# Sinkhorn routing inside an attention-and-experts kernel: partition sums by all-ones matmuls on TensorE in place of GpSimd's reduce

## What is computed

```python
x = window_attention(q, k, v)              # 4 x 8 heads, 576 positions, width 64, window 64 -> [2304, 512]
logits = x @ w_gate                        # [2304, 8]
P = np.exp(logits - logits.max())
for _ in range(8):
    P /= P.sum(1, keepdims=True) + 1e-09   # sums over the 8 experts
    P /= P.sum(0, keepdims=True) + 1e-09   # sums over all 2304 tokens
    P *= N / E
for e in range(8):
    out += P[:, e:e + 1] * (np.maximum(x @ w1[e], 0.0) @ w2[e])
```

## Time and profile before

| | us |
|---|---|
| median of 3 executions (lowest to highest) | 1751.09 (1749.76 to 1754.01) |
| the profiled execution, its own time | 1752.63 |
| its span in the trace | 1750.8 |
| PE busy | 1633.5 |
| POOL busy | 998.6 |
| DVE busy | 725.3 |
| ACT busy | 525.8 |

### The profile page before, as it was taken

One profiled execution on the slowest core, in us unless ns is written; L12 is line 12 of the kernel. 1 busy time (PEld: TensorE's weight loads), 2 busy tenths in 40 slices (PEclk: granted clock), 3 DMA queues, 4 the chain that ended last, 5 costly groups with the idle time before them and its releaser, 6 DMA issues.

```text
span 1750.8 us, 23864 instructions
## 1 busy us (share of the span) xinstructions
PE 1633.5 (93%) x8652; PEld 1465.1 (84%) x8652; DVE 725.3 (41%) x1260; ACT 525.8 (30%) x751; POOL 998.6 (57%) x654
## 2 busy tenths in 40 slices
PE   6878453999999999999999999999999999999999
PEld 6777342888888888898888888898888888898888
DVE  4563212444344344344434434434433443443443
ACT  2332001323333233432333323333333332333332
POOL 5662121666555667766655566567865556655562
PEclk8988775999999999999999999999999999999999
DMA  7841000221122211132112221121311121112210
GB/s 224 239 132 41 8 24 24 72 73 72 48 72 72 72 68 52 72 109 73 64 56 72 72 72 60 60 72 72 108 57 64 72 72 72 52 68 72 72 60 36
DMA packets 35432, 129.17 MB, mean 74 GB/s; under 512 B 4288, under 2 KB 4416, under 8 KB 35392
## 3 DMA queue, kind: packets, MB, share of 16 engines
q1 hardware_dynamic: 35392, 128.65, 21.5%
HBM read 123.91 MB, written 4.72 MB: 73 GB/s over the span
## 4 chain that ended last, share of the span: by engine, by line
PE 85%; issue 7%; DMA 3%; POOL 2%; DVE 1%; SPq 0%; ACT 0%; POOLq 0%; DVEq 0%
PE ps L393 15%; PE ps L394 15%; PE ps L392 15%; PE ps L376 13%; PE ps L372 13%; PE ps L374 13%; DMA qk_buf<-qk 3%; PE ps L289 1%; POOL w_lo L602 1%; PE ps L310 1%; POOL w_lo L609 1%; PE ps L320 1%; DVE xv_lo L751 0%; DVE p_t L730 0%; PE ps L300 0%
## 5 line engine op out<-in xcount | busy, mean ns | idle before, releaser
L602 POOL TENSOR_TENSOR w_lo<-w_raw,w_hi 128x1792 fp32r<-128x1792 f32 (+1 forms) x102 | 391.4, 3838 | 524.6 <-ACT w_hi L446 495.3
L372 PE MATMUL ps<-xv_hi,w_hi 128*128 128x384 f32 x1344 | 456.5, 340 | 70.7 <-DVE h_lo L757 38.3
L488 ACT ACTIVATE h_hi<-ps 128x384 fp32r<-128x384 f32 x384 | 189.0, 492 | 983.4 <-DVE ps L775 448.2
L392 PE MATMUL ps<-w_hi,h_hi 128*128 128x512 f32 x1152 | 457.4, 397 | 10.9 <-POOL w_lo L609 10.9
L393 PE MATMUL ps<-w_lo,h_hi 128*128 128x512 f32 x1152 | 459.3, 399 | 0.0
L394 PE MATMUL ps<-w_hi,h_lo 128*128 128x512 f32 x1152 | 458.2, 398 | 0.0
L376 PE MATMUL ps<-xv_hi,w_lo 128*128 128x384 f32 x1344 | 456.9, 340 | 0.0
L374 PE MATMUL ps<-xv_lo,w_hi 128*128 128x384 f32 x1344 | 454.4, 338 | 0.0
L757 DVE SCALAR_TENSOR_TENSOR h_lo<-ps,h_hi 128x384 fp32r<-128x384 f32 x384 | 214.2, 558 | 390.8 <-ACT h_hi L488 390.8
L372 PEld LDWEIGHTS ps<-xv_hi,w_hi 128*128 128x128 f32 x1344 | 256.6, 191 | 104.3 <-DVE h_lo L757 26.6
L374 PEld LDWEIGHTS ps<-xv_lo,w_hi 128*128 128x128 f32 x1344 | 256.6, 191 | 28.8
(11 more groups left out here) (59 smaller groups left out, 962.9 us busy)
## 6 DMA issues: line engine op xcount, KB each, us to landing
w_raw<-w SPq DMA_DIRECT2D x192, 512.0 KB, 3.9
qk_buf<-qk SPq DMA_DIRECT2D x16, 864.0 KB, 7.2
v_win<-v SPq DMA_DIRECT2D x16, 288.0 KB, 4.1
out<-x_raw SPq DMA_DIRECT2D x18, 256.0 KB, 3.4
v_win<-v SPq DMA_DIRECT2D x16, 256.0 KB, 5.1
const_sb<-consts SPq DMA_DIRECT2D x1, 160.0 KB, 4.7
wg<-w_gate SPq DMA_DIRECT2D x1, 16.0 KB, 10.5
```

Of the source, the lines that this page charges most:

```text
L372: nc.tensor.matmul(o, w1_hi[:, slot, c], xv_hi[:, at, kk, :], start=(opens and kk == 0), stop=False, skip_group_check=not opens)
L392: nc.tensor.matmul(ps_y[t], h_hi[slot][:, f, c], w2_hi[slot][:, f, :], start=opens, stop=False)
L488: nc.scalar.activation(h_hi[slot][:, f, half * HT:(half + 1) * HT], o, ACT.Relu)\
L602: last = nc.gpsimd.tensor_tensor(w1_lo[:, slot, c], w1_raw[:, slot, (lo + 1) * BLK:(hi + 1) * BLK], w1_hi[:, slot, c].bitcast(F32), ALU.su ...
```

## The change

The nine reduces of POOL go. A matrix `ones` (128 x 128) is the stationary operand of a matmul whose moving operand is `col_part` (8 columns); every partition of the result then holds the column sums. For the maximum, DVE multiplies the identity matrix by each partition's maximum (`max_diag`), the same matmul puts all 128 maxima on every partition, and DVE takes the maximum along them. The results lie in the 128 columns of the two product banks that the products leave free (`spread`). In steps 2 and 3 PE has such a matmul behind P6, P7 and P4, and waits before P7 and before P5 until DVE has read the last one out of the bank in which that product begins. DVE has the turns at three other places of its window. POOL has its ordinary window in steps 1 to 3. Four windows of PE are written out where a loop ran them. `const_sb`, which holds the identity, lives on past attention. The cut diff:

```diff
+        spread = [ps[:, 512 * i + HT:512 * (i + 1)] for i in range(2)]
...
+            def spread_max(at):
+                pe.wait_ge(ones_set, 1)
+                pe.wait_ge(max_part_ready, 1)
+                nc.tensor.matmul(spread[at], ones[:], max_diag[:], start=True, stop=True).then_inc(max_spread, 1)
+
+            def spread_columns(i, at):
+                pe.wait_ge(col_part_ready, i + 1)
+                nc.tensor.matmul(spread[at][:, 0:E], ones[:], col_part[:], start=True, stop=True)\
+                  .then_inc(col_sum_ready, 1)
...
                 for k, (lo, hi) in enumerate([(0, 2), (2, 4), (4, 6), (6, 8), (8, 10), (10, 11), (11, 12)]):
-                    multiply(s, first, n, j % 2, k)
+                    if top and k == P7:
+                        pe.wait_ge(max_all_ready, 1)
+                    if after_p6 is not None and k == P7:
+                        pe.wait_ge(chain, after_p6 * 8 + 5)
+                    if after_p7 is not None and k == P5:
+                        pe.wait_ge(chain, after_p7 * 8 + 5)
+                    multiply(s, first, n, slot, k)
+                    if top and k == P6:
+                        spread_max(1 - slot)
+                    if after_p6 is not None and k == P6:
+                        spread_columns(after_p6, 1 - slot)
+                    if after_p7 is not None and k == P7:
+                        pe.wait_ge(h_ready, n * 4 + 1)
+                        spread_columns(after_p7, slot)
+                    if after_p4 is not None and k == P4:
+                        spread_columns(after_p4, 1 - slot)
...
+                if s == 0:
+                    for j in range(FP):
+                        window(s, False, FP + j, j, TT - (2 * TT if j == 0 else TT), after_p6=None if j else 7)
+                with pe.Fori(1 if s else 2, E) as e:
...
-            pool.wait_ge(max_part_ready, 1)
-            nc.gpsimd.partition_all_reduce(max_all[:], max_part[:], P, RMAX).then_inc(max_all_ready, 1)
...
-                reduce_columns(3 * n - 5)
...
+            for n in (1, 2, 3):
+                window(n, n, landed(n + 2))
...
+                if after_p6 is not None:
+                    dve.wait_ge(col_sum_ready, after_p6 + 1)
+                if top:
+                    dve.wait_ge(max_spread, 1)
                 add_u2(n, slot)
+                if top:
+                    shift_logits(1 - slot)
+                if after_p6 is not None:
+                    read_columns(after_p6, 1 - slot)
+                    columns(after_p6)
+                    if not last:
+                        row_sums(after_p6 + 1)
+                        rows(after_p6 + 1)
                 some(0, 1)
                 rest(n, slot, bank[slot], 0, 0, 0)
...
                 add_u3(n, slot)
+                if after_p7 is not None:
+                    read_columns(after_p7, slot)
+                    columns(after_p7)
+                    row_sums(after_p7 + 1)
+                    rows(after_p7 + 1)
...
                 rest(n, slot, bank[slot], 1, 1, 1)
+                if after_p4 is not None:
+                    read_columns(after_p4, 1 - slot)
                 add_c21(n, slot)
+                if after_p4 is not None:
+                    columns(after_p4)
                 rest(n, slot, bank[1 - slot], 1, 0, 2)
                 add_c12(n, slot)
+                if after_p4 is not None:
+                    row_sums(after_p4 + 1)
                 rest(n, slot, bank[slot], 0, 1, 3)
+                if after_p4 is not None:
+                    rows(after_p4 + 1)
...
+                nc.vector.tensor_scalar(max_diag[:], ident, max_part[:, 0:1], None, ALU.mult)\
+                nc.vector.tensor_reduce(max_all[:], spread[at], AX_X, ALU.max).then_inc(max_all_ready, 1)
+                nc.vector.tensor_scalar(col_sum[:], spread[at][:, 0:E], EPS, None, ALU.add).then_inc(chain, 1)
```

More of the change, by code:

```diff
@@ L89, in build @@
         max_all = sb(ctx, "max_all", [P, 1])
+        max_diag = sb(ctx, "max_diag", [P, P])
+        ones = sb(ctx, "ones", [P, P])
+        const_sb = sb(ctx, "const_sb", [P, WINDOW + 2 * P])
         w2_hi = [sb(ctx, "w2_hi0", [P, 2, DM], F32R)]
@@ L429, in _ @@
                     n = s * PER_SB + j
-                    if n:
-                        window(s, s and j == 0, n, j, None if n == 1 else n // FP * TT - 2 * TT)
-                with pe.Fori(1, E) as e:
+                    taken = None if n == 1 else n // FP * TT - 2 * TT
+                    if n == 1:
+                        window(s, False, n, j, taken, True, after_p4=0)
+                    elif n in (2, 3):
+                        window(s, False, n, j, taken, False, 3 * n - 5, 3 * n - 4, 3 * n - 3)
+                    elif n:
+                        window(s, j == 0, n, j, taken)
+                if s == 0:
+                    for j in range(FP):
+                        window(s, False, FP + j, j, TT - (2 * TT if j == 0 else TT), after_p6=None if j else 7)
+                with pe.Fori(1 if s else 2, E) as e:
                     for j in range(FP):
@@ L843, in rows @@
                 nc.vector.tensor_reduce(row_sum[:], prob[:], AX_X, ALU.add).then_inc(chain, 1)
-                dve.wait_ge(chain, c + 1)
+                dve.wait_ge(chain, i * 8 + 1)
                 nc.vector.tensor_scalar(row_sum[:], row_sum[:], EPS, None, ALU.add).then_inc(chain, 1)
+            def rows(i):
+                c = i * 8
                 dve.wait_ge(chain, c + 2)
@@ L866, in columns @@
                 dve.wait_ge(chain, c + 8)
-            def turn(i):
-                columns(i)
-                rows(i + 1)
             nc.vector.memset(p_t[:], 0.0).then_inc(warm_ready, 1)
+            nc.vector.memset(ones[:], 1.0).then_inc(ones_set, 1)
             nc.vector.memset(ps_s[:, 0, 0:WINDOW], NEG).then_inc(pads_set, 1)
@@ L904, in _ @@
             rest(0, 0, bank[0], 0, 1, 3)
-            window(1, 1, None, shift_logits, lambda: rows(0), lambda: turn(0))
-            window(2, 2, None, lambda: turn(1), lambda: turn(2), lambda: turn(3))
-            window(3, 3, None, lambda: turn(4), lambda: turn(5), lambda: turn(6))
-            columns(7)
+            window(1, 1, None, True, after_p4=0)
+            window(2, 2, None, False, 1, 2, 3)
+            window(3, 3, None, False, 4, 5, 6)
             for s in range(SB):
```

49 lines of the change are left out of this document (18 added, 31 removed).

## The result

The changed kernel takes **1672.56 us** (median of 4 runs, 1666.65 to 1673.12). The kernel before took 1752.55 us (4 runs, 1749.76 to 1755.45) beside it. The ratio is 0.9538 (95% interval 0.951 to 0.9566), 80 us less. The forecast was 1652, with a range of 1647 to 1663: direction and cause of the gain hold, the size is 20 us off. The profiled execution took 1672.8 us, its span is 1671.0.

What follows compares the result with a forecast made beforehand. POOL's idle around nine reduces was taken to hold up DVE and PE: 1752.63 - 101.67 excess + 1.8 for small matmuls = 1652.8, or 1651.2 against the median; forecast 1652 us, range 1647 to 1663.

Steps and rivals of the forecast that it cites:

- What bounds the kernel: From about 149 to 309 us POOL's nine all-reduces bring 125 us of idle, 13.9 us a piece; DVE and PE wait.
- the idle isn't the reduces': Rival: the 7.3 us behind each reduce belong to POOL's hand-over to ordinary work, so 66 us stay; 1699 us, chance 0.03.
- The excess, 101.67 us,: From u2 of step 1 to u2 of step 5: 164.42 us against 62.75 for four undisturbed steps; all to be gained.
- The small matmuls: Nine float32 matmuls added to PE, 0.20 us each, 1.8 us in all; bounds 0 and 4.5 us.
- The sum that the prediction worked out by that rule: Four passes at 0.10 us a record: nine small matmuls 3.6 us, the sum 1.8 us more; not adopted.
- DVE's turns moved: DVE's 2.46 us turns at three places of a step, costed at nothing as covered by PE; uncovered, eight cost 19.7 us.
- sign of being wrong there: The DVE step is wrong if PE waits for h_lo by more than 1 us a step.
- DVE becomes late: Rival: hand-overs of some 0.1 us use up the 0.4 us slack; half the turns 1662, all 1672; chance 0.14.
- the third place: DVE's last turn place in a step: third rest ends near 12.3, next P1 needs it at 12.75; slack 0.4 us, smallest.
- the second place: Turn behind u3, ending near 8.0: second rest ends near 10.35, P3 needs it at 11.0; slack 0.7 us.
- The clock rival: Rival: PE's clock falls between hand-overs at every small matmul, some 1.7 us each, +15 us, 1667; chance 0.06.
- the dear matmuls: Small matmuls at the upper bound of 0.5 us a piece, 4.5 us for nine; counted in the range's upper end.

Runs made afterwards that it cites:

- the layout's: Kernel before with only the changed kernel's buffers: const_sb lives on, ones and max_diag allocated, ones set by DVE; 1754.08 us, ratio 0.9998.
- POOL's work cut: Changed kernel with POOL's subtractions and sums for the weights of steps 2 to 5 on eight columns only; 1660.93 us, ratio 0.9476.
- the two later profiles: Changed kernel run twice more, unaltered; 1670.26 us (6 runs, ratio 0.9522) and 1670.07 us (one run).
- the idle bank's kernel: Changed kernel with turn operands in PSUM, both constants left out, the turn behind u3 keeping its sums in the other product bank; 1657.92 us, ratio 0.9446.
- the one with the extra addition: Kernel with turn operands in PSUM plus one eight-column DVE addition behind u2: both inputs in SBUF in step 2, one in PSUM in step 3; 1668.63 us.
- operand in PSUM: Changed kernel with turn sums and reciprocals in PSUM, maximum in ACT's bias, both constants left out, u3 behind the turn; 1661.60 us, ratio 0.9469.
- no constant on the row sums: Changed kernel without DVE's addition of 1e-9 to the row sums; 1670.58 us, ratio 0.9531.

## Why the prediction was wrong in size

**What bounds the kernel** held. The 125 us of idle on POOL were the reduces': the changed kernel has no idle from "issue" on POOL from 149 to 220 us, and one reduce put back brought back 12.8 us of it. The rival that the idle isn't the reduces' falls with that.

**The excess, 101.67 us,** was right for the profile that it was read from. That one execution was not a typical one: in the two other profiles of the kernel before and in the layout's the excess is 97.7 to 99.2 (160.4 to 161.9, less 62.75). Its attention was early (u2 of step 1 at 153.47, the others' at 156.7 to 158.7), and the median behind it, 1751.09, was 3.9 us below that of 17 later runs. By the siblings the sum is 1755.0 - 97.7 + 1.7 = 1659.0 us, or 1657.5 with 99.2: 6 to 7 us of the miss, in the starting time and in the excess together. The kernel in which nothing that PE waits for is held, with POOL's work cut, measured 1660.93.

**The small matmuls,** 9 x 0.20 = 1.8 us, measured 1.74, two records each, 0.23 a piece in a step. The Trainium skill, "FP8 and Floating Point Precision", in its notes on TensorE, gives a true float32 matmul four passes. The sum that the prediction worked out by that rule, 1.8 us more, is not borne out.

**"DVE's turns moved" is the step that failed.** The prediction said: "Nothing in it is new except that the sums come out of PSUM", and cost the turns at nothing. A turn of 2.46 us was timed while POOL stood idle in its reduces. In the changed kernel the turn behind u2 runs beside POOL's w1_rest and w2_rest, and lasts from 178.65 to 185.88, 7.2 us. The prediction's own sign of being wrong there, PE waiting for h_lo by more than 1 us a step, came true with 3.28. Two things were missed:

- what POOL does during the turn in its new place. The prediction moved POOL's work earlier and DVE's turns elsewhere, and never laid the two beside each other.
- when the first rest is due. I took P5, at 6.2 us of the step. The change makes the small matmul behind P7 wait for that rest (`h_ready` in the diff), which is at 4.9 us. The rest ended at 8.2 (186.35 - 178.18), and PE stood for 3.28. With an unheld turn the rest would have been in time for either (3.9 by the prediction); with the held one it would have missed P5 too, by some 2 us (8.2 - 6.2, an estimate).

The rival "DVE becomes late", at 0.14, had place and price nearly right, but gave as its cause hand-overs of 0.1 us and named the third place as the tightest; there nothing was late, and at the second place only in step 1, where in the two later profiles PE stands 0.5 and 1.0 us ahead of P3. Its 1672 for all turns agrees with the measurement by accident: one turn a step is held for long, in steps 2 to 4, and PE pays for two of them, 5 to 6 us each, not for eight at 2.46. The range's upper end was also loosely added: the dear matmuls and half the turns on 1652 give 1664.7, not 1663, and the lower end, 1749.76 - 101.67, is 1648, not 1647.

**The clock rival** (0.06) happened as a consequence. The small matmuls alone bring no fall: with them and no stand the clock is 1.00 in all four steps, with POOL's work cut and in the idle bank's kernel. Behind the stand of 3.28 us PE goes on at a granted clock of 0.50 for 5.9 us. By stretch, in step 2 of the changed kernel, before the stand and after it:

```profile
178.18:183.12 4.94, 4.94 (x24) 4.09 (x23) 4.73 (x6) 1.43 (x2) 4.55 (x2) 1.00 0.00 0
186.40:192.30 5.90, 5.90 (x16) 5.16 (x17) 3.12 (x10) 0.00 (x0) 1.03 (x2) 0.50 0.38 152
```

A clock of 0.50 (1.2 GHz) over 5.90 us costs 3.0 us: 16.35 + 3.28 + 3.0 = 22.6, the measured 22.64. In step 3 it is 21.46 - 16.35 - 3.28 = 1.8 us: behind a stand of the same length the clock is low for a shorter time, and in the two later profiles both steps are like this one (21.43 to 21.46 us, clock 0.92). So of the 11.9 us in this profile 6.6 are the stands and 4.8 the clock; the rest is in step 1.

**The closing sum** is 1755.0 - 97.7 + 1.74 + 11.5 = 1670.5 us, the 11.5 being 75.98 - 64.49; measured were 1670.26 and 1672.56. The 97.7 is the lowest excess of the four profiles; with 99.2 the sum is 1669.0.

**What stays open** is the start. The u2 of step 1 lies between 151.4 and 166.4 us in the changed kernels and between 153.5 and 158.7 in those with the old order. The transfers of attention (the qk loads) take 6.6 to 8.7 us in the median from profile to profile. The start goes with them: the idle bank's kernel has the shortest loads and starts first, the one with the extra addition has the longest and starts last. The mean clock from 5 to 110 us lies between 0.84 and 0.92. So the new order doesn't force a late start, and the layout alone shows no cost. But the ten profiles of changed kernels start at 159.3 us in the mean and the four with the old order at 156.5, and the closing sum leaves up to 3.6 us. Whether the change itself delays the start by so much these runs can't tell.

## What to carry to other kernels

When a change moves a small instruction, look up what the neighbouring engine runs at the new place, and treat a duration measured beside an idle POOL as valid only there: an 18-column addition cost 0.18 us in one place and 2.24 in the other. Where a short chain on DVE has to run beside long elementwise work of POOL, keep one operand of each of its instructions in PSUM, and clear the whole chain, since the wait moves to the next instruction that can be held. Read excess and starting time from several profiles before claiming a forecast to 1%: here one profile and the median beside it were 6 to 7 us out.

## What the runs showed of the hardware

- A DVE instruction with two SBUF inputs that started beside POOL's w1_rest or w2_rest ended with it, even one on 8 columns (2.56 us), and the profile books the wait as its duration. One input in PSUM lifts it (0.16 us).
- Not all of DVE's SBUF work is held: beside w1_rest a reciprocal took 0.20 us (changed kernel) and a reduction of 144 columns 0.30 (operand in PSUM), though both read and write SBUF, while adding a constant to 18 columns beside w2_rest took 2.24.
- One reduce put back on POOL brought 12.8 us of idle (5.90 ahead, 6.89 behind) for 0.38 us of work; a small matmul in place of a column sum adds 0.23 us to a step.
- After a stand of 3.28 us the granted clock was 0.50 for 5.9 us of busy PE in one step, nearly doubling the price of the wait; in the other steps of the changed kernel with such a stand the fall cost 1.8 us. With stands of 2.6 us (no constant on the row sums) the clock fell in one step and not in the other.
